# Attention and mixer on one core: query tiles shifted by one 64-block, and the scores of a head in one group

## The reference

```python
scores = scale * np.matmul(q, k.transpose(0, 1, 3, 2))
mask = block_i >= block_j                      # blocks of 64
scores = np.where(mask, scores, -1000000000.0)
scores = scores - np.max(scores, axis=-1, keepdims=True)
attn = np.exp(scores)
attn = attn / (np.sum(attn, axis=-1, keepdims=True) + 1e-09)
x = np.matmul(attn, v)                         # heads side by side: (B, S, 512)

h = np.maximum(x @ w_in, 0.0)                  # 1024 columns: u, v
v_n = (v - mu) / np.sqrt(var + 1e-06)
v_s = np.einsum('ts,bsd->btd', w_spatial, v_n) + b_spatial[None, :, None]
x = (u * v_s) @ w_out

xn = (x - mu) / np.sqrt(var + 1e-06) * g_ln
out = x + np.maximum(xn @ w_ch1, 0.0) @ w_ch2  # 512 to 2048 to 512
```

## Time and profile before

| | us |
|---|---|
| median of 3 runs | 792.93 |
| lowest, highest | 792.04, 794.08 |
| the profiled execution | 791.29 |
| its span | 789.5 |
| granted TensorE clock | 1.00 |
| TensorE busy | 778.3 |
| VectorE busy | 497.2 |
| ScalarE busy | 380.5 |
| GpSimd busy | 394.4 |

### The profile page before, as it was taken

The page is one execution under the profiler, slowest core; times in us unless marked ns, Lnnn a source line. Parts: engine busy times, 40 slices in busy tenths (PEclk is TensorE's granted clock), DMA queues, the critical chain, the costliest instruction groups (busy, mean ns, idle before and its releaser), DMA issues.

```text
span 789.5 us, 14255 instructions
## 1 busy us (share of the span) xinstructions
PE 778.3 (99%) x5088; PEld 669.1 (85%) x5088; DVE 497.2 (63%) x1028; ACT 380.5 (48%) x970; POOL 394.4 (50%) x508
## 2 busy tenths in 40 slices
PE   8999999999999999999999999999999999999998
PEld 6767888778887788879988989988898889898987
DVE  7886746366563665528767776688656687545445
ACT  5996675456564565524353333443342345333431
POOL 4886655334353243503356455656454556554541
PEclk9999999999999999999999999999999999999999
DMA  6453332312123220041263231003100000300002
GB/s 233 149 177 95 113 103 77 102 58 72 54 73 102 71 68 25 1 135 53 69 195 112 68 119 54 28 1 120 54 27 1 1 1 33 129 0 1 1 1 81
DMA packets 38149, 56.40 MB, mean 71 GB/s; under 512 B 3136, under 2 KB 20544, under 8 KB 38080
## 3 DMA queue, kind: packets, MB, share of 16 engines
q1 hardware_dynamic: 38080, 55.49, 21.5%
HBM read 46.04 MB, written 9.44 MB: 70 GB/s over the span
## 4 chain that ended last, share of the span: by engine, by line
PE 87%; DVE 6%; ACT 4%; issue 3%; POOL 0%; ACTq 0%; POOLq 0%; DVEq 0%
PE psum L1391 24%; PE psum L1392 23%; PE psum L1393 23%; PE psum L1312 5%; PE psum L1357 4%; ACT probs L808 3%; PE psum L1372 2%; DVE neg_max L1035 2%; PE psum L1377 2%; PE psum L1473 1%; DVE mix_buf L1110 1%; PE psum L1443 1%; PE psum L1426 0%; PE psum L1424 0%; DVE stats L1089 0%
## 5 line engine op out<-in xcount | busy, mean ns | idle before, releaser
L759 POOL TENSOR_TENSOR wp_r<-block,wp_r 128x256 fp32r<-128x256 f32 x168 | 133.7, 803 | 168.3 <-ACT wp_r L941 166.0
L1216 DVE TENSOR_TENSOR sums<-psum,sums 128x384 f32<-128x384 f32 x216 | 113.6, 554 | 105.8 <-PE psum L1393 105.1
L969 ACT ACTIVATE h_r<-sums 128x384 fp32r<-128x384 f32 x96 | 50.4, 526 | 228.8 <-PE psum L1393 119.1
L691 POOL TENSOR_SCALAR probs<-probs,row_inv 128x512 f32<-128x512 f32 (+4 forms) x160 | 92.5, 593 | 108.5 <-DVE row_inv L1048 108.5
L1035 DVE TENSOR_REDUCE neg_max<-psum 128x1 f32<-128x512 f32 (+4 forms) x160 | 80.7, 538 | 58.1 <-PE psum L1312 57.0
L1393 PE MATMUL psum<-w_r,h_r 128*128 128x512 f32 x288 | 114.2, 397 | 0.0
L1392 PE MATMUL psum<-w_r,h_r 128*128 128x512 f32 x288 | 113.7, 395 | 0.0
L1391 PE MATMUL psum<-operand,wp_r 128*128 128x384 f32 x336 | 113.2, 337 | 0.2 <-DVE sums L1216 0.2
L1392 PE MATMUL psum<-operand,wp_r 128*128 128x384 f32 x336 | 113.0, 336 | 0.0
L1393 PE MATMUL psum<-operand,wp_r 128*128 128x384 f32 x336 | 112.4, 334 | 0.0
L808 ACT ACTIVATE probs<-psum,neg_max 128x512 f32<-128x512 f32 (+4 forms) x160 | 89.9, 567 | 45.8 <-DVE neg_max L1035 43.6
(11 more groups left out here) (119 smaller groups left out, 1614.0 us busy)
## 6 DMA issues: line engine op xcount, KB each, us to landing
qk_raw<-qk SPq DMA_DIRECT2D x32, 576.0 KB, 4.0
...
```

Of the source, the lines that this page charges most:

```text
L691: pool.tensor_scalar(probs[:, n % 2, c], probs[:, n % 2, c], row_inv[:, n % 2, AT[t]:AT[t] + 1], 1.0, ALU.mult, ALU.mult).then_inc(normed, 1)
L759: pool.tensor_tensor(wp_lo[:, n % WP], w1[i % BLOCKS][:, WEIGHT[j]], wp_hi[:, n % WP].bitcast(F32), ALU.subtract).then_inc(wp_lo_done, 1)
L1216: dve.tensor_tensor(dst, product_bank(i, j), other, ALU.add).then_inc(c_summed, 1)
```

## The change

The query tiles are cut anew: the first (tile 0, now called `OWN`) has only the first block of 64 queries, and tiles 1 to 4 have 128 queries each, from query 64, 192, 320 and 448 on. `KEYS` becomes 64, 192, 320, 448, 576: 1600 columns a head. Each tile of 128 queries now ends with two blocks, of which the second sees one block more.

- The transposes of tiles 1 to 4 are t full ones each, ten in all. What is left over, the last key block of each tile, and tile 0, is made by five 64x64 transposes from the upper rows (tile `OWN`), into rows 0 to 63 of the output.
- Scores of tiles 1 to 4 are made by one group of ten matmuls, `score_head`, in step 0, in banks 0 to 2. The order pairs LOW with HIGH rows; a block of more than 512 keys is cut in two. In the middle the group waits for its own first two matmuls of tile 2. Tile 0's single matmul, `score_first`, stands behind the transposes of step 2, in bank 4 up to head 8 and in bank 5 after.
- Maxima and exponentials follow: four tiles in step 0, tile 0 in step 2. ACT's `output_right` stands ahead of its copies, DVE's copy of tile 2 ahead of the maximum of tile 0. Step 0 transposes tiles 4, 3 and 1, step 2 tile 2 and `OWN`.
- `attend(n)` also waits for all exponentials of head n + 1.
- POOL's weight splits stand in step 0, behind `scale_q`, from round 8 on (before in step 1, behind `normalise`).
- In batches 0 and 2 the empty mixer slot moves from the end of the batch to the middle of its last round.

```diff
@@ -66,7 +66,9 @@
-    KEYS = [min(P * (t + 1), S) for t in range(NT)]
+    KEYS = [BLOCK + P * t for t in range(NT)]
+    QUERY_AT = [0] + [BLOCK + P * (t - 1) for t in range(1, NT)]
@@ -324,70 +328,52 @@
-        DVE_TILES, ACT_TILES = [3, 1], [0, 2, 4]
+        OWN = 0
+        DVE_TILES, ACT_TILES = [4, 2], [3, 1, OWN]
         SPLIT_Q = 392
...
         def transposed_free(pe, n, t):
...
-            elif t == 1:
+            if t == 2 and n >= H:
                 pe.wait_ge(t_copied_dve, len(DVE_TILES) * n + 1)
...
-        TILES = [3, 0, 2, 1, 4]
-        PEAKS = {3: 1, 0: 3, 2: 3, 1: 5, 4: 5}
+        TILES = [4, 3, 1, 2, 0]
         AT = [TILES.index(t) for t in range(NT)]
-        MADE = {3: 1, 0: 3, 2: 3, 1: 4, 4: 5}
-        FIRST = 3
+        FIRST, TURNED = 4, 3
...
         def score_of(n, t):
+            flat = psum.rearrange("p a n -> p (a n)")
             if t == 0:
...
+                return (m_bank[:, 1, :] if n <= H else o_bank)[BLOCK:P, 7 * BLOCK:8 * BLOCK]
+            start = {4: 0, 3: KEYS[4], 2: KEYS[4] + KEYS[3], 1: KEYS[4] + KEYS[3] + KEYS[2]}[t]
+            return flat[:, start:start + KEYS[t]]
...
+        SPARE = sum(len(r) for r in GROUP_STEPS[:H - 1])
@@ -396,7 +382,10 @@
-            return [(at // GROUPS, at % GROUPS)] if at >= 0 and in_batch(at // GROUPS, at % GROUPS) else []
+            b, g = at // GROUPS, at % GROUPS
+            if b % 2 == 0 and g >= SPARE:
+                return [(b, g - 1)] if g > SPARE else []
+            return [(b, g)] if at >= 0 else []
...
@@ -739,10 +735,12 @@
+                        for i in pieces_at(n - 1) if n >= H else []:
+                            split_piece(i)
                     elif step == 1 and n + 1 < HEADS:
                         for t in TILES[:FIRST]:
                             normalise(n + 1, t)
-                        for i in pieces_at(n - 1):
+                        for i in pieces_at(n - 1) if n < H else []:
...
@@ -899,15 +892,15 @@
-                        copy_transposed(n, 0)
-                        copy_transposed(n, 2)
                         if n >= 1:
                             output_right(n - 1)
+                        copy_transposed(n, 3)
+                        copy_transposed(n, 1)
                     elif step == 1:
                         for b, k in x_split_at(n, 1):
                             split_x(b, k)
                     elif step == 2:
-                        copy_transposed(n, 4)
+                        copy_transposed(n, OWN)
@@ -1029,12 +1021,14 @@
-                dve.wait_ge(scored_first if t in TILES[:FIRST] else scored_second, 4 * (n + 1))
+                if t == 0:
+                    dve.wait_ge(scored_own, n + 1)
+                else:
+                    dve.wait_ge(scored_wide if t in WIDE else scored_narrow, SCORES * (n + 1))
...
@@ -1124,10 +1117,11 @@
-                        invert(n, 1)
+                        if n >= 1:
+                            invert(n, 1)
                         if n >= 1:
                             output_left(n - 1)
-                        copy_transposed(n, 3)
+                        copy_transposed(n, 4)
@@ -1137,10 +1131,10 @@
+                        copy_transposed(n, 2)
                         if n + 1 < HEADS:
                             for t in TILES[FIRST:]:
                                 max_tile(n + 1, t)
-                        copy_transposed(n, 1)
@@ -1312,50 +1306,50 @@
...
+            def seen(n, t, half, upper, start=0, end=512):
+                query = QUERY_AT[t] // BLOCK + upper
+                keys = slice(start, min(BLOCK * (query + 1), end))
+                return score(n, score_of(n, t)[HIGH if upper else LOW, keys], half, query, keys)
+            def score_head(n):
+                pe.wait_ge(q_scaled, n + 1)
+                if n >= 1:
+                    pe.wait_ge(exped, NT * (n - 1) + FIRST)
+                seen(n, 2, HIGH, 1, end=256).then_inc(scored_narrow, 1)
+                seen(n, 4, LOW, 1).then_inc(scored_wide, 1)
+                seen(n, 2, HIGH, 0).then_inc(scored_narrow, 1)
+                seen(n, 4, LOW, 0).then_inc(scored_wide, 1)
+                seen(n, 3, HIGH, 0).then_inc(scored_wide, 1)
+                seen(n, 3, HIGH, 1).then_inc(scored_wide, 1)
+                pe.wait_ge(scored_narrow, SCORES * n + 2)
+                seen(n, 1, LOW, 0).then_inc(scored_narrow, 1)
+                seen(n, 2, LOW, 1, start=256).then_inc(scored_narrow, 1)
+                seen(n, 1, LOW, 1).then_inc(scored_narrow, 1)
+                seen(n, 4, HIGH, 1, start=512, end=KEYS[4]).then_inc(scored_wide, 1)
             def score_first(n):
...
+                pe.wait_ge(exped, NT * n)
                 if n > H:
...
+                    pe.wait_ge(o_right_done, n - 1)
+                score(n, score_of(n, 0), LOW, 0, slice(0, BLOCK)).then_inc(scored_own, 1)
...
+                if t != OWN:
+                    for j in range(t):
+                        c = P_AT[t] + P * j
+                        last = pe.transpose(place[:, P * j:P * (j + 1)], probs[:, n % 2, c:c + P], ident[:, :])
+                else:
+                    for j in range(NT):
+                        c = P_AT[j] + P * j
+                        last = pe.transpose(place[:, BLOCK * j:BLOCK * (j + 1)], probs[HIGH, n % 2, c:c + BLOCK],
+                                            ident[HIGH, HIGH])
@@ -1367,6 +1361,7 @@
+                pe.wait_ge(exped, NT * min(n + 2, HEADS))
@@ -1443,25 +1438,25 @@
...
                     if step == 0:
                         if n + 1 < HEADS:
-                            score_first(n + 1)
+                            score_head(n + 1)
                         if n >= 1:
                             attend(n - 1)
-                        for t in TILES[:FIRST]:
+                        for t in TILES[:TURNED]:
                             transpose_tile(n, t)
                     elif step == 2:
+                        for t in TILES[TURNED:]:
+                            transpose_tile(n, t)
                         if n + 1 < HEADS:
-                            score_second(n + 1)
-                        for t in TILES[FIRST:]:
-                            transpose_tile(n, t)
+                            score_first(n + 1)
                     for b, g in groups_at(n, step):
                         mixer(b, g)
             attend(HEADS - 1)
```

132 lines of the change are left out of this document (41 added, 91 removed).

## The result

The changed kernel takes 802.58 us (median of four runs, 801.74 to 805.67) against 792.55 us of the kernel before in the same comparison: ratio 1.0136, interval 1.0118 to 1.0155. It is 1.4% slower where 1.3% faster was forecast, and far outside the range. The profiled execution took 801.74 us, its span is 799.9.

What follows compares the result with a forecast made beforehand. Bound: softmax engines and TensorE in one loop before the mixer, TensorE from 90.41 to 345.24 us. Gains 1.9 + 1.2 + 0.9 + 5.0 + 1.0 + 0.1 = 10.1 us: 781.2 profiled, 782.8 forecast, range 779.5 to 788.7.

Steps and rivals of the forecast that it cites:

- The in-group wait: Inside the new score group TensorE waits for its first two HIGH matmuls; cost nothing, 0.2 us a head if signalled late.
- T+0.7: With T the score group's start, the two awaited matmuls done at 0.7 us, while the low half streams until 0.9.
- Rival (b): The in-group wait or late maxima cost 0.2 us a head, giving 788.7 us; chance 10%.
- tile 2's wait for VectorE's copy of tile 4: Tile 2's transposes, n >= 8: copy at T+5.3 (T: score group's start), TensorE there at T+5.6; free, 0.3 us left.
- the mixed rounds: From 90.41 to 345.24 us: 20 rounds with scores gain 0.25 each, 5.0 us, and three stalls of 0.33 go, 1.0.
- Heads without mixer: Seven rounds before the mixer, looped through GpSimd's normalisation and the own tile: 5.2 us each, ending at 51.4; 1.9 us gained.
- The start of head 2: Longer start-up, twice scores, maximum and four exponentials at 4.75 us: with signals 15.0 us instead of 14.45.
- the stalls of the earlier trace: Score groups waiting for exponentials, 1.47, 0.86 and three of 0.33 us; all 3.3 us were to go.
- rival (a): The five own 64x64 transposes are slow, 0.3 us a head in 31 heads, 9 us: 791.5 us; chance 6%.
- The weight splits: Three GpSimd splits ahead of the rstd, round from 79.36 us: VectorE later, a u group's bank freed 0.45 us late.
- attend's new wait: attend(n-1) waits for all exponentials of head n; tile 0's covered by a mixer group of 1.7 us or more.
- the round at 53.31: First round with mixer groups, 12.36 us before: 11.2 forecast, 1.2 us gained (0.9 to 1.6).

Runs made afterwards that it cites:

- e2: The changed kernel with the wait inside the score group put directly behind its two matmuls of tile 2, instead of four matmuls later; 818.6 us (one run).
- e7: The changed kernel with tile 2's two awaited matmuls issued one behind the other, ahead of the 512-column matmul of tile 4 that stood between them; 794.26 us, ratio 1.0018.
- e1: The changed kernel with the last 64 columns of tile 4 scored ahead of the wait inside the score group instead of behind it; 794.16 us, ratio 1.0012.
- e4: The changed kernel with ScalarE's output_right put behind its two copies of step 0 again; 796.69 us, ratio 1.0050.
- v2_all: The changed kernel with e7's order, tile 4's last 64 columns ahead of the wait, output_right behind ScalarE's two copies, and 14 warm-up matmuls for 6; 785.85 us.
- v3: v2_all with GpSimd's weight splits behind the normalisation of the next head again in all rounds; 788.96 us, ratio 0.9945.

## Why the prediction was wrong

**The in-group wait** is the step that failed, "Cost: nothing". The columns were counted right: 1.44 us forecast, 1.45 measured once the wait costs nothing, 0.26 and 0.25 for tile 0. For the two matmuls alone my T+0.7 was near: the wait ends at T+0.74 where nothing stands between them (e2). What I didn't see is that the second is counted only after the 512-column matmul of tile 4 that the program puts ahead of it, so the wait is over only at T+1.18, while the low half is empty from T+0.93. Rival (b) named the wait and priced it at 0.2 a head if the signal were late: it costs 0.33, by this order and not by a slow signal, and e7, which swaps the two lines, gets 8.3 us back. It fell on two more places that I had put no price on: VectorE's maxima hang on the matmul behind the wait (e1: 8 us for that line), and ScalarE's copies hang on these.

**What stands behind the wait in step 2.** I followed tile 2's wait for VectorE's copy of tile 4, forecast it for T+5.3, and took 0.3 us of slack. That was near: T+5.4 in the round from 109.48, and TensorE waited for it in two rounds only, 58.20 and 84.96 (1.9 us in all in the view of waits). But the own tile's transposes wait for ScalarE's copies of the tiles 3 and 1 in the same way, and these stand behind four exponentials and `output_right`, at T+6.6. The text lists the move of `output_right` ahead of these copies, and the prediction never costs it. The wait costs some 4 us in the mixed rounds, and with the group at 1.45 us it is there still (6.4 us in 14 places in e7); e4 takes it away.

**Heads without mixer**, "5.2 us". I summed one loop, through GpSimd and the own tile, and took the busy time of the others as cover. The loop that closes is scores, two maxima, four exponentials, scores. From my own numbers it gave 1.69 to the maxima, 1.35 for two of them (1,024 columns, as the three of the earlier trace rows), 2.3 and 0.1: 5.4, already more than the 5.2, if I had seen that the first exponential waits for two maxima (tile 4 reaches into tile 3's bank). With the wait it is 5.74, without its cost 5.34 to 5.43. The start of head 2 is 3.55 us later than before, where I had 0.55: 5.74 us from head 0 to head 1 and 6.2 to head 2 instead of 4.75 each, a first score 0.68 later, and in the second of them the clock.

**Right**: the stalls of the earlier trace rows are gone: no score group of the mixed rounds waits for an exponential, and the mixer groups ahead of these scores, 4.22 and 3.69 us long with the stall in them, take 3.3 to 3.4; one change of shape less saves 0.09 (a 14-matmul group ahead of step 2 takes 1.94 us instead of 2.03). Better than forecast are the step-2 transposes: 0.31 + 0.39 = 0.70 us where nothing waits, against 0.81, so rival (a) was wrong in its sign. The Trainium skill, page TensorEngine Tiling (Array Packing), section Restrictions, says that column tiling disables transpose mode for FP32 input; five own transposes in 0.39 us, 0.06 us apart and with one record each, don't show it. The same page of the Trainium skill says, in the section Gotcha 1: PSUM Pressure, that different row tiles can't access the same PSUM bank simultaneously. That is why the wait exists; no run here leaves it out while two halves share a bank, so no run tests the rule.

**The weight splits** were priced at 0.45 us by a u group's bank. The changed kernel loses 0.16 us ahead of attend and 0.29 us for that bank in the round from 96.89 us: 0.45 in all, of which only the second is what I described. That the splits cause either isn't shown, so the agreement is luck. In v2_all, where TensorE comes earlier, attend's new wait, which I had called covered, is 0.92 us. There the sign of the term is the other way: with the move taken back v2_all loses 1.7 us, and the bank's wait grows to 1.40 (v3). On the changed kernel itself the move wasn't tried alone.

**Where the 20.5 us went** between the forecast for the profiled execution (781.2 us) and its 801.74, by the spans: the start 3.0, seven rounds at 5.74 instead of 5.2 us 3.8, the round at 53.31 1.9 (13.08 instead of 11.2), the next two 1.8 (25.61 instead of 23.84), the mixed rounds 10.3 (260.68 instead of 250.4, that is 256.37 less the 6.0 forecast), and 0.3 back after them.

Two sums of the prediction are slightly off and change nothing: seven rounds of 5.45 us from 15.0 gain 0.2 us and not 0.5, and rival (a), 9 us above 782.8, is 791.8.

With the lines that cause the waits put right, and 14 warm-up matmuls, the kernel has the forecast's sign and most of its size: v2_all at 785.85 us stands in the range of 779.5 to 788.7, and its mixed rounds take 250.2 us, where the sum had 250.4. That doesn't mend the prediction, which was of the kernel as written.
